# Another order for batch 0's attention and first products, and output products that wait for their low halves apart

## The chip, the cores and the metric

The kernel runs on one core of a Trainium2 chip. The metric is the device time of one execution in microseconds, measured over whole executions. The core's engines are called PE (TensorE, matmuls; PEld are its weight loads), DVE (VectorE), ACT (ScalarE), POOL (GpSimd) and SP (SyncE, which here only issues transfers).

## What is computed

Three stages follow each other on 4 batches of 768 tokens. All inputs are float32.

```python
# attention with decay: 8 heads, head_dim 48, state 48 x 48 per head
for t in range(S):
    state = alpha[:, :, t, :, None] * state + einsum('bhd,bhe->bhde', k[:, :, t], v[:, :, t])
    y[:, :, t] = einsum('bhd,bhde->bhe', q[:, :, t], state)
# x: the heads side by side, (4, 768, 384)
# first MLP with a spatial gate
h = gelu_tanh(x @ w_in)                       # 384 -> 1024
u, v = h[..., :512], h[..., 512:]
v_n = (v - mean(v)) / sqrt(var(v) + 1e-6) * g_ln
v_s = einsum('ts,bsd->btd', w_sg, v_n) + b_sg[None, :, None]
x = x + (u * v_s) @ w_out                     # 512 -> 384
# Fourier mixing and second MLP
u = x + real(fft(fft(x, axis=1), axis=2))
un = (u - mean(u)) / sqrt(var(u) + 1e-6)
out = u + relu(un @ w_ch1) @ w_ch2            # 384 -> 1536 -> 384
```

## The kernel before, in words

**Products in two halves.** A float32 product is made of three fp32r matmuls: each operand is split into a high half (written by ACT as a cast) and a low half (the rest, written by DVE as a difference), and PE adds high x high, high x low and low x high into one PSUM bank. `product(dst, terms)` (L1212 to L1219, its matmul is L1218) does this for a list of terms, in that order, term by term. Every matmul is preceded by its own weight load.

**How the program is written.** Each engine has its own queue of steps in an order written out by hand as lists of pairs ("step", index). Engines meet only through counting semaphores: a step waits until another engine's count is reached. An engine never goes past a step that waits.

**The opening (batch 0's attention and first products).** The lists `FIRST_DVE`, `FIRST_ACT`, `FIRST_POOL` and `FIRST_PE` (L73 to L96) order it. The tokens are six chunks (or tiles) of 128; the steps are:

- "prep" c and "query" c on DVE: two scans over the decays of chunk c (`rev` L953, `fwd` L965), each with a product into the decayed keys `kd` (L959) and queries `qu` (L969). The inputs of a chunk (`decay_k_q`) come by one transfer of 674 KB.
- "scores" c: PE transposes the keys (L1239) and multiplies keys by queries (L1251); DVE masks the result into `sm` (L983); ACT copies the keys by token into `kn` (L767).
- "out" c: PE makes the chunk's new state (L1273, for chunks 1 and 2 with the decayed state added by L1267) and its output (L1283, L1288); ACT copies the output to `y_by_token` (L770); for chunks 3 and 4 DVE keeps the state (L994) and "carry" decays it (L977); for chunks 1 to 3 "decay" on ACT does both (L781, L784).
- "x" t: PE transposes output tile t (L1320), ACT writes its high half `x_hi` (L797), DVE its low half `x_lo` (L1023).
- "v" t and "u" i: 6 products of 9 matmuls of 128x512 and 8 of 9 matmuls of 128x384 with the two halves of `w_in`. ACT applies the gelu (L803, L811). For v, DVE takes the statistics (L1032), POOL the reciprocal root `rs` (L649, L652), DVE normalizes (L999, "norm" below), ACT and DVE write the halves `vn_hi`, `vn_lo` (L790, L1004). "v" t on DVE also normalizes tile t-1 and writes the low half of tile t-2; "v end" does the last ones. v t needs the halves of x t and piece 0 of the weights, u i needs three tiles of x (0 to 2 for even i, all six for odd i) and piece 1.
- "next ..." are the first steps of batch 1's attention, made inside the opening.

`FIRST_PRODUCTS` is the order of u and v on PE. The products before index `FIRST_ROLLED`, and that one, all use bank 4, so each waits for the gelu of the one before; from `FIRST_ROLLED` + 1 on they roll over four banks, and wait until all of batch 0's attention is done (`wait_first_bank`, L1294 to L1303).

**The weight pieces.** The weights come as 12 pieces of 128x1536 in float32, through two raw buffers in the opening. Pieces 0 and 1 are `w_in`, 2 is `w_out`, 3 to 5 are `w_sg`. "split" n is ACT's high half (L755) and DVE's low half (L933). For pieces 2, 3 and 4 the low half is made otherwise: ACT writes the negated high half ("neg", L760) and POOL issues a transfer that adds the raw piece to it ("sum", L659). A piece's transfer (L526) is issued by SP when the piece before it in the same buffer has been read; SP's order is: chunks 0 to 3, pieces 0, 1, chunks 4, 5, pieces 2, 3, chunk 0 of batch 1, pieces 4, 5. Split 3 on ACT also waits for the whole of batch 0's attention, since `w_sg` lies over its buffers.

**The spatial stage.** After the opening, `phase1` runs for each batch: 8 spatial products s ("s" i, 18 matmuls of 128x384 with `w_sg`), each gated on DVE (L1063, L1067), split by ACT (`gated_hi`, L834) and DVE (`gated_lo`, L1009), and 8 output steps ("o" j, `output`, L1367 to L1378): three token tiles of 3 matmuls each with `w_out`, added up in three banks over four steps. The first spatial product of batch 0, `w_sg_hi` in the profile, waits for all halves of v, all gelus of u, and the low halves of pieces 2 to 5. The attention of the next batch runs beside it.

**The last stage.** `phase2` runs for each batch: 24 hidden steps "h" k (9 matmuls with `w_c1`; ACT writes `hidden_hi`, L885, DVE `hidden_lo`, L1165) and 24 output steps "o" k, each queued two hidden steps behind (`LAG = 2`), in two halves of 12 steps. An output step (L1480 to L1500) has 9 matmuls, 3 for each of three token tiles, into the banks `ACC`. After 12 steps "fin" on DVE adds each bank into `u_kept` (L1178) and counts `fin_done` once for each tile; the first output step of the next half waits for all three. The Fourier mixing of the next batch runs beside it.

## Time and profile before

| | |
|---|---|
| median of 3 runs (lowest, highest) | 710.98 us (709.78, 711.03) |
| the profiled execution | 710.78 us |
| its span, first to last instruction | 708.9 us |
| PE, PEld, DVE, ACT, POOL busy | 99%, 94%, 63%, 29%, 11% |
| mean granted TensorE clock | 0.998 |
| opening, to the first spatial product | 0 to 70.6 us |
| spatial stages of four batches | 70.6 to 376 us |
| last stage of four batches | 376 to 709 us |

The profiled execution's time is 1.9 us above its span: that is what lies around the first and the last instruction. All times inside the kernel are microseconds from the span's start. A matmul's listed duration overlaps the next one's, since they are pipelined; how fast PE goes is read from the distance of two starts. An idle time in brackets says how long the engine stood still before the instruction, and what ended it.

### The profile page before, as it was taken

What the parts mean: (1) busy time and instruction counts of PE and PEld (TensorE: products, weight loads), DVE (VectorE), ACT (ScalarE), POOL (GpSimd) and SP (SyncE); (2) the same over time, 40 slices, a digit from 0 to 9 for tenths busy, and PEclk for the clock granted to TensorE, in tenths of its full rate; (3) what the DMA queues carried; (4) which work ended last, traced back from release to release, by engine and by line L of the source; (5) the groups of instructions that cost most, each with busy time, mean ns of one, the idle gap of its engine ahead of it and who ended that gap; (6) DMA issues with size and microseconds to landing.
All of it is one profiled execution on the core that took longest, in us unless ns stands there. A gap on an engine that the chain in (4) does not pass through costs nothing.

```text
span 708.9 us, 13451 instructions
## 1 busy us (share of the span) xinstructions
PE 698.5 (99%) x5572; PEld 667.2 (94%) x5572; DVE 446.5 (63%) x859; ACT 204.3 (29%) x390; POOL 80.9 (11%) x125
## 2 busy tenths in 40 slices
PE   7999999999999999999999999999999999999998
PEld 6789999899998999989999999999999999999998
DVE  7997887996768967669587746381634726331212
ACT  2647111341114411144336222232221322222111
POOL 1022000120002100051211203001300201000000
PEclk9999999999999999999999999999999999999999
DMA  9757223322222131071346312012300200000000
GB/s 287 224 140 185 83 71 97 122 52 81 72 84 85 52 101 52 35 214 44 113 124 210 103 35 79 1 37 65 89 24 33 59 8 33 0 35 1 15 19 34
DMA packets 21358, 56.69 MB, mean 80 GB/s; under 512 B 2404, under 2 KB 14824, under 8 KB 21304
## 3 DMA queue, kind: packets, MB, share of 16 engines
q1 hardware_dynamic: 18104, 44.53, 20.3%
q0 software_dynamic: 3056, 11.26, 6.3%
q8 instruction: 40, 0.66, 0.4%
q10 hardware_dynamic: 144, 0.13, 0.1%
q14 instruction: 14, 0.11, 0.0%
HBM read 46.45 MB, written 9.46 MB: 79 GB/s over the span
## 4 chain that ended last, share of the span: by engine, by line
PE 92%; DVE 5%; DMA 2%; issue 1%; ACT 0%; SPq 0%; DVEq 0%; ACTq 0%
PE bank L1218 79%; PE bank L1251 3%; PE bank L1288 3%; PE bank L1283 2%; PE bank L1320 1%; PE bank L1438 1%; PE bank L1273 1%; PE bank L1239 1%; PE bank L1452 1%; DMA raw_weights_a<-in_w_second 1%; DVE u_kept L1178 1%; DMA decay_k_q<-in_akq 1%; DVE fwd L965 1%; DVE fwd_b L965 1%; DVE rev_b L953 1%
## 5 line engine op out<-in xcount | busy, mean ns | idle before, releaser
L1218 PE MATMUL bank<-ut_hi,w_c 128*128 128x384 f32 x576 | 162.8, 338 | 0.3 <-DVE hidden_lo L1165 0.3
L1165 DVE SCALAR_TENSOR_TENSOR hidden_lo<-bank,hidden_hi 128x384 fp32r<-128x384 f32 x96 | 53.4, 556 | 158.2 <-ACT hidden_hi L885 157.7
L1218 PEld LDWEIGHTS bank<-ut_hi,w_c 128*128 128x128 f32 x576 | 105.4, 188 | 1.2 <-DVE hidden_lo L1165 0.7
L885 ACT ACTIVATE hidden_hi<-bank 128x384 fp32r<-128x384 f32 x96 | 47.2, 492 | 199.5 <-PE bank L1218 199.2
L1218 PE MATMUL bank<-w_c_hi,hidden_hi 128*128 128x384 f32 x288 | 96.7, 336 | 0.5 <-DVE u_kept L1178 0.5
L1218 PE MATMUL bank<-ut_lo,w_c 128*128 128x384 f32 x288 | 96.3, 334 | 0.0
L1218 PE MATMUL bank<-w_c_hi,hidden_lo 128*128 128x384 f32 x288 | 96.3, 334 | 0.0
L1218 PE MATMUL bank<-w_c_lo,hidden_hi 128*128 128x384 f32 x288 | 96.2, 334 | 0.0
L1218 PE MATMUL bank<-w_sg_hi,vn_hi 128*128 128x384 f32 x192 | 66.2, 345 | 0.0
L1218 PE MATMUL bank<-w_sg_hi,vn_lo 128*128 128x384 f32 x192 | 64.2, 334 | 0.0
L1218 PE MATMUL bank<-w_sg_lo,vn_hi 128*128 128x384 f32 x192 | 64.2, 334 | 0.0
L834 ACT CAST gated_hi<-gated 128x384 fp32r<-128x384 f32 x32 | 16.4, 513 | 139.8 <-DVE gated L1067 139.8
L1218 PEld LDWEIGHTS bank<-w_c_hi,hidden_hi 128*128 128x128 f32 x288 | 54.1, 188 | 1.6 <-issue 1.6
L1218 PEld LDWEIGHTS bank<-ut_lo,w_c 128*128 128x128 f32 x288 | 54.2, 188 | 0.0
L1218 PEld LDWEIGHTS bank<-w_c_lo,hidden_hi 128*128 128x128 f32 x288 | 54.1, 188 | 0.0
L1218 PEld LDWEIGHTS bank<-w_c_hi,hidden_lo 128*128 128x128 f32 x288 | 54.1, 188 | 0.0
L1218 PEld LDWEIGHTS bank<-w_sg_hi,vn_hi 128*128 128x128 f32 x192 | 36.0, 188 | 1.6 <-issue 0.2
L1218 PEld LDWEIGHTS bank<-w_sg_lo,vn_hi 128*128 128x128 f32 x192 | 36.1, 188 | 0.0
L1218 PEld LDWEIGHTS bank<-w_sg_hi,vn_lo 128*128 128x128 f32 x192 | 36.0, 188 | 0.0
L1218 PE MATMUL bank<-w_out_hi,gated_hi 128*128 128x384 f32 x96 | 33.1, 345 | 0.4 <-DVE gated_lo L1009 0.4
L1218 PE MATMUL bank<-x_hi,w_in_hi 128*128 128x384 f32 x96 | 32.9, 342 | 0.0
L1218 PE MATMUL bank<-x_hi,w_in_lo 128*128 128x384 f32 x96 | 32.2, 335 | 0.0
(200 smaller groups left out, 1333.2 us busy)
## 6 DMA issues: line engine op xcount, KB each, us to landing
decay_k_q<-in_akq SPq DMA_DIRECT2D x19, 673.8 KB, 5.0
x_scratch<-x_half SPq DMA_DIRECT2D x8, 579.0 KB, 4.6
out_tiles<-u_kept SPq DMA_DIRECT2D x24, 192.0 KB, 2.0
values<-in_v SPq DMA_DIRECT2D x18, 192.0 KB, 5.1
x_quarters<-x_scratch SPq DMA_DIRECT2D x16, 168.9 KB, 3.2
raw_first_a<-in_w_first SPq DMA_DIRECT2D x3, 768.0 KB, 11.4
raw_first_b<-in_w_first SPq DMA_DIRECT2D x3, 768.0 KB, 4.7
raw_weights_b<-in_w_second SPq DMA_DIRECT2D x3, 768.0 KB, 5.3
```

The costliest lines, as they stand in the source:

```text
L834: nc.scalar.copy(gs[0][:, i % 3, :], gt[:, i % 3, :]).then_inc(ghi_done, 1)
L885: nc.scalar.activation(hid[0][:, i % 4, :], HB[i % 2][:, 0:HS], ACT.Relu).then_inc(hhi_done, 1)
L953: nc.vector.tensor_tensor_scan(rev[:, NA - 2::-1], raw[:, NA - 1:0:-1], resets[:, NA - 1:0:-1], 1.0, ALU.mult, ALU.add).then_inc(rev_done, 1)
L965: nc.vector.tensor_tensor_scan(fwd[:], raw[:, 0:NA], resets[:], 0.0, ALU.mult, ALU.add).then_inc(fwd_done, 1)
L1165: nc.vector.scalar_tensor_tensor(out=hid[1][:, i % 4, :], in0=HB[i % 2][:, 0:HS], scalar=0.0, in1=f32(hid[0][:, i % 4, :]), op0=ALU.max, o ...
L1178: nc.vector.tensor_tensor(ub[:, HT * i + j, :], ACC[j][:, 0:DM], ub[:, HT * i + j, :], ALU.add).then_inc(fin_done, 1)
L1218: ins = nc.tensor.matmul(dst, a, c, start=start and n == 0, stop=stop and n == len(passes) - 1)
L1239: ins = nc.tensor.transpose(ky[:, g * PR:(g + 1) * PR], kd[:, g, :], ident[0:PR, 0:PR])
L1251: ins = nc.tensor.matmul(sc[j][:, g * P:(g + 1) * P], kd[at, g, :], qu[at, g, :], start=True, stop=True)
L1273: ins = nc.tensor.matmul(sc[0][at, cols], kn[:, g, at], values[:, cols], start=not adds, stop=True, skip_group_check=True)
L1283: nc.tensor.matmul(ky[q, g * PP:(g + 1) * PP], qu[:, g, q], std[:, c % 2, g, :], start=True, stop=False, skip_group_check=True)
L1288: ins = nc.tensor.matmul(ky[q, h * D:(h + 1) * D], sm[:, g, j, q], values[:, h * D:(h + 1) * D], start=c == 0, stop=True, skip_group_check ...
```

## The change

It has two parts.

1. The four lists of the opening are written in another order, with `FIRST_ROLLED` at "v" 2 instead of "v" 3. No step is added or removed, and the code that carries the steps out is as it was. The pieces' transfers keep their places in SP's program; what they wait for (split 0, split 1, the high halves of pieces 2 and 3) stands elsewhere in the lists of ACT and DVE, and the sums of pieces 2 and 3 stand elsewhere in POOL's.
2. A new helper `tile_products` makes an output step of three token tiles: for each tile high x high and high x low of the weights, then a wait, then for each tile low x high. Before, the whole step waited for the low half of its operand; now it waits for the high half at its start (`ghi_done`, `hhi_done`) and for the low half before its last three matmuls (`glo_done`, `hlo_done`). It is used for the 32 output steps of the spatial stage and for the last stage's, but for the first of each half and the last two of all. The first output step of each half (f == 0) keeps the old order and waits for the sum of each tile by itself.

```diff
--- before.py
+++ after.py
@@ -71,28 +71,28 @@
 
 
 FIRST_DVE = ([("prep", 0), ("query", 0), ("prep", 1), ("scores", 0), ("query", 1), ("prep", 2)]
-             + [("scores", 1), ("query", 2), ("prep", 3), ("query", 3), ("scores", 2), ("split", 0)]
-             + [("x", 0), ("split", 1), ("scores", 3), ("prep", 4), ("x", 1), ("query", 4), ("out", 3)]
-             + [("x", 2), ("scores", 4), ("carry", 4), ("prep", 5), ("out", 4), ("query", 5), ("carry", 5)]
-             + [("v", 0), ("next prep", 0), ("x", 3), ("scores", 5), ("v", 1), ("x", 4), ("v", 2)]
-             + [("next query", 0), ("v", 3), ("x", 5), ("next scores", 0), ("v", 4), ("v", 5), ("split", 5)]
-             + [("v end", 0), ("v end", 1)])
-FIRST_ACT = ([("scores", 0), ("decay", 1), ("out", 0), ("scores", 1), ("scores", 2), ("decay", 2)]
-             + [("out", 1), ("scores", 3), ("split", 0), ("split", 1), ("x", 0), ("decay", 3), ("out", 2)]
-             + [("x", 1), ("split", 2), ("neg", 2), ("x", 2), ("v", 0), ("scores", 4), ("out", 3), ("x", 3)]
-             + [("u", 2), ("out", 4), ("v", 1), ("u", 4), ("scores", 5), ("x", 4), ("v", 2), ("out", 5)]
-             + [("split", 3), ("v", 3), ("neg", 3), ("next scores", 0), ("x", 5), ("split", 4), ("v", 4)]
-             + [("neg", 4), ("u", 6), ("v", 5), ("u", 0), ("split", 5), ("u", 3), ("u", 5), ("v end", 0)]
-             + [("u", 1), ("v end", 1), ("u", 7)])
-FIRST_POOL = ([("sum", 2), ("v", 0), ("v", 1), ("v", 2), ("sum", 3), ("v", 3), ("sum", 4), ("v", 4)]
+             + [("scores", 1), ("query", 2), ("x", 0), ("split", 0), ("prep", 3), ("scores", 2)]
+             + [("query", 3), ("split", 1), ("x", 1), ("prep", 4), ("scores", 3), ("query", 4), ("prep", 5)]
+             + [("x", 2), ("query", 5), ("out", 3), ("carry", 4), ("scores", 4), ("scores", 5), ("out", 4)]
+             + [("carry", 5), ("x", 3), ("v", 0), ("next prep", 0), ("x", 4), ("v", 1), ("next query", 0)]
+             + [("v", 2), ("x", 5), ("v", 3), ("v", 4), ("next scores", 0), ("v", 5), ("v end", 0)]
+             + [("v end", 1), ("split", 5)])
+FIRST_ACT = ([("scores", 0), ("out", 0), ("decay", 1), ("scores", 1), ("x", 0), ("split", 0)]
+             + [("decay", 2), ("out", 1), ("scores", 2), ("split", 1), ("v", 0), ("x", 1), ("scores", 3)]
+             + [("out", 2), ("split", 2), ("decay", 3), ("v", 1), ("x", 2), ("out", 3), ("scores", 4)]
+             + [("u", 4), ("neg", 2), ("u", 2), ("x", 3), ("scores", 5), ("out", 4), ("split", 3), ("x", 4)]
+             + [("out", 5), ("neg", 3), ("v", 2), ("split", 4), ("x", 5), ("v", 3), ("neg", 4), ("v", 4)]
+             + [("u", 0), ("v", 5), ("split", 5), ("u", 6), ("v end", 0), ("u", 7), ("v end", 1), ("u", 3)]
+             + [("next scores", 0), ("u", 5), ("u", 1)])
+FIRST_POOL = ([("v", 0), ("sum", 2), ("sum", 3), ("v", 1), ("v", 2), ("v", 3), ("sum", 4), ("v", 4)]
               + [("v", 5)])
-FIRST_PE = ([("scores", 0), ("out", 0), ("scores", 1), ("out", 1), ("scores", 2), ("scores", 3)]
-            + [("x", 0), ("out", 2), ("x", 1), ("v", 0), ("out", 3), ("x", 2), ("scores", 4), ("u", 2)]
-            + [("x", 3), ("out", 4), ("v", 1), ("scores", 5), ("u", 4), ("x", 4), ("v", 2), ("out", 5)]
-            + [("v", 3), ("x", 5), ("u", 6), ("next scores", 0), ("v", 4), ("u", 0), ("v", 5), ("u", 3)]
-            + [("u", 5), ("u", 1), ("u", 7)])
+FIRST_PE = ([("scores", 0), ("out", 0), ("x", 0), ("scores", 1), ("out", 1), ("scores", 2), ("v", 0)]
+            + [("x", 1), ("out", 2), ("scores", 3), ("v", 1), ("x", 2), ("out", 3), ("scores", 4)]
+            + [("u", 4), ("x", 3), ("scores", 5), ("u", 2), ("out", 4), ("out", 5), ("x", 4), ("v", 2)]
+            + [("v", 3), ("v", 4), ("x", 5), ("next scores", 0), ("v", 5), ("u", 0), ("u", 6), ("u", 7)]
+            + [("u", 3), ("u", 5), ("u", 1)])
 FIRST_PRODUCTS = [step for step in FIRST_PE if step[0] in ("u", "v")]
-FIRST_ROLLED = FIRST_PRODUCTS.index(("v", 3))
+FIRST_ROLLED = FIRST_PRODUCTS.index(("v", 2))
 FIRST_U = [i for step, i in FIRST_PRODUCTS if step == "u"]
 
 
@@ -1218,6 +1218,16 @@
                     ins = nc.tensor.matmul(dst, a, c, start=start and n == 0, stop=stop and n == len(passes) - 1)
                 return ins
 
+            def tile_products(dsts, x, w, lo_done, start, stop):
+
+                for dst, hi in zip(dsts, x[0]):
+                    nc.tensor.matmul(dst, hi, w[0], start=start, stop=False)
+                    nc.tensor.matmul(dst, hi, w[1], start=False, stop=False)
+                pe.wait_ge(*lo_done)
+                for dst, lo in zip(dsts, x[1]):
+                    ins = nc.tensor.matmul(dst, lo, w[0], start=False, stop=stop)
+                return ins
+
             def keep_warm(dst, times):
 
                 for _ in range(times):
@@ -1366,15 +1376,14 @@
 
             def output(b, j):
                 f = j % 4
-                pe.wait_ge(glo_done, 8 * b + j + 1)
+                pe.wait_ge(ghi_done, 8 * b + j + 1)
                 if j == 0:
                     pe.wait_ge(ug_done, 8 * (b + 1))
                 if j == 4:
                     pe.wait_ge(x1a_done, 2 * b + 1)
-                for t in range(HT):
-                    ins = product(GB[2 + t][:, 0:DM],
-                                  [([x[:, j % 3, t * P:(t + 1) * P] for x in gs],
-                                    [w[:, f, :] for w in w_out])], start=f == 0, stop=f == 3)
+                ins = tile_products([GB[2 + t][:, 0:DM] for t in range(HT)],
+                                    [[x[:, j % 3, t * P:(t + 1) * P] for t in range(HT)] for x in gs],
+                                    [w[:, f, :] for w in w_out], (glo_done, 8 * b + j + 1), f == 0, f == 3)
                 ins.then_inc(po_done, 1)
 
             def phase1(b, attends):
@@ -1479,24 +1488,31 @@
                             product(HB[i % 2][:, 0:HS], terms).then_inc(hid_done, 1)
                     elif step == "o":
                         h, f = i // NF, i % NF
-                        pe.wait_ge(hlo_done, 2 * NF * b + i + 1)
                         if f * DM % PIECE == 0 and isinstance(b, int) and b == 0:
                             wait_lo(pe, NP1 + KD + f * DM // PIECE)
                             pe.wait_ge(x1a_done, 2 * B)
-                        if f == 0:
-                            need(pe, fin_done, NT * b + HT * h)
                         if isinstance(b, int) and b == B - 1 and i >= 2 * NF - 2:
                             if i == 2 * NF - 1:
+                                pe.wait_ge(hlo_done, 2 * NF * b + i + 1)
                                 for j in range(HT):
                                     product(ACC[j][:, 0:DM],
                                             [([x[:, n % 4, j * P:(j + 1) * P] for x in hid],
                                               [w[:, n % NF, :] for w in w_c2]) for n in (i - 1, i)],
                                             start=False).then_inc(o_tile_done, 1)
                             continue
-                        for j in range(HT):
-                            ins = product(ACC[j][:, 0:DM],
-                                          [([x[:, i % 4, j * P:(j + 1) * P] for x in hid],
-                                            [w[:, f, :] for w in w_c2])], start=f == 0, stop=f == NF - 1)
+                        if f == 0:
+                            pe.wait_ge(hlo_done, 2 * NF * b + i + 1)
+                            for j in range(HT):
+                                need(pe, fin_done, NT * b + HT * (h - 1) + j + 1)
+                                ins = product(ACC[j][:, 0:DM],
+                                              [([x[:, i % 4, j * P:(j + 1) * P] for x in hid],
+                                                [w[:, f, :] for w in w_c2])], stop=False)
+                        else:
+                            pe.wait_ge(hhi_done, 2 * NF * b + i + 1)
+                            ins = tile_products([ACC[j][:, 0:DM] for j in range(HT)],
+                                                [[x[:, i % 4, j * P:(j + 1) * P] for j in range(HT)] for x in hid],
+                                                [w[:, f, :] for w in w_c2], (hlo_done, 2 * NF * b + i + 1), False,
+                                                f == NF - 1)
                         ins.then_inc(o_done, 1)
 
             pe.wait_ge(std_zeroed, 1)
```

## Rows read from the trace of the kernel before

**Rows 1.** Busy time by stretch: us, busy of each engine (instructions), PE clock, DMA, GB/s.

```profile
24.00:28.00 4.00, 4.00 (x41) 2.71 (x39) 3.52 (x5) 3.00 (x3) 0.00 (x0) 0.58 0.51 143
...
47.10:69.20 22.10, 22.10 (x166) 19.63 (x168) 17.26 (x37) 16.20 (x24) 6.91 (x12) 1.00 0.63 148
...
376.00:709.00 333.00, 329.11 (x2085) 324.98 (x2083) 147.32 (x295) 83.86 (x161) 32.44 (x40) 1.00 0.14 44
```

**Rows 2.** Timeline of DVE in the opening: start, us, engine, line, operation, out<-in.

```profile
19.46 0.06 DVE L950 MEMSET resets<- 112x4 f32 x1
...
25.28 1.76 DVE L933 TENSOR_TENSOR w_in_lo<-raw_first_a,w_in_hi 128x1536 fp32r<-128x1536 f32 x1 [0.48 <-ACT w_in_hi L755]
...
34.94 0.55 DVE L994 TENSOR_TENSOR state<-bank,state_decayed 112x384 f32<-112x384 f32 x1
...
35.40 0.55 DVE L1023 TENSOR_TENSOR x_lo<-bank,x_hi 128x384 fp32r<-128x384 f32 x1
...
38.25 0.06 DVE L950 MEMSET resets<- 112x4 f32 x1
...
40.22 0.55 DVE L994 TENSOR_TENSOR state<-bank,state_decayed 112x384 f32<-112x384 f32 x1
...
46.36 0.55 DVE L1023 TENSOR_TENSOR x_lo<-bank,x_hi 128x384 fp32r<-128x384 f32 x1
```

**Rows 3.** Timeline of PE in the opening.

```profile
34.59 0.55 PE L1239 MATMUL bank<-constants,kd 112*128 112x112 f32 x4
...
36.17 0.44 PE L1218 MATMUL bank<-x_hi,w_in_hi 128*128 128x384 f32 x1
...
37.85 0.49 PE L1320 MATMUL bank<-constants,y_by_token_even 128*128 128x128 f32 x3
...
38.27 0.56 PE L1273 MATMUL bank<-values_first,kn 128*48 128x48 f32 x16
...
40.37 0.50 PE L1218 MATMUL bank<-w_in_hi,x_hi 128*128 128x512 f32 x1
...
47.06 0.52 PE L1320 MATMUL bank<-constants,y_by_token_even 128*128 128x128 f32 x3 [1.11 <-DVE x_lo L1023]
...
70.58 0.44 PE L1218 MATMUL bank<-w_sg_hi,vn_hi 128*128 128x384 f32 x1
```

**Rows 4.** What PE waited for: us in total, times, longest.

```profile
PE bank L1218 <- DVE u_kept L1178: 0.5, 3, 0.2
```

**Rows 5.** Timeline of PE and DVE between two halves of the last stage.

```profile
508.87 0.33 PE L1218 MATMUL bank<-w_c_hi,hidden_lo 128*128 128x384 f32 x1
509.05 0.33 PE L1218 MATMUL bank<-ut_hi,w_c 128*128 128x384 f32 x1
...
509.31 1.49 DVE L1178 TENSOR_TENSOR u_kept<-bank,u_kept 128x384 f32<-128x384 f32 x3 [0.55 <-PE bank L1218]
...
510.43 0.34 PE L1218 MATMUL bank<-ut_hi,w_c 128*128 128x384 f32 x1
510.95 0.41 PE L1218 MATMUL bank<-w_c_hi,hidden_hi 128*128 128x384 f32 x1 [0.18 <-DVE u_kept L1178]
511.20 0.33 PE L1218 MATMUL bank<-w_c_lo,hidden_hi 128*128 128x384 f32 x1
```

**Rows 6.** Timeline of PE and ACT at output steps and at the last stage's start.

```profile
124.31 0.44 PE L1218 MATMUL bank<-w_out_hi,gated_hi 128*128 128x384 f32 x1 [0.18 <-DVE gated_lo L1009]
...
373.80 0.44 PE L1218 MATMUL bank<-w_out_hi,gated_hi 128*128 128x384 f32 x1 [0.22 <-DVE gated_lo L1009]
...
377.26 1.48 ACT L755 CAST w_c_hi<-raw_weights_a 128x1536 fp32r<-128x1536 f32 x1 [2.73 <-DMA raw_weights_a<-in_w_second]
...
379.77 0.44 PE L1218 MATMUL bank<-ut_hi,w_c 128*128 128x384 f32 x1 [0.34 <-DVE hidden_lo L1165]
```

**Rows 7.** Instructions on `w_sg_lo`, 61 to 63 us: sum 4's issue and landing.

```profile
L659 POOL DMA_DIRECT2D w_sg_lo<-in_w_first x1: 883/883/883, 62.1 to 62.1; - x1
...
DMA to landing us min/median/max: 7.6/7.6/7.6
```

## The prediction

> **What bounds the kernel now.** I read the busy table by stretch first, then the two timelines of the opening batch, then the waits of TensorE (PE). From 47 us on PE is the bound: it is busy 22.10 of the 22.10 us up to 69.20, and 329.11 of the last 333 us, at a granted clock of 1.00 [rows 1]. Ahead of that VectorE (DVE) is the bound: between 19.46 and 35.40 us its steps stand end to end with one idle spell of 0.48 us [rows 2]. PE's last long wait there is 1.11 us, for DVE's `x_lo` of token tile 3, and from 47.06 us it runs unbroken to the first spatial product at 70.58 us [rows 3]. So time is won in two ways only: reach the point from which PE never waits with less PE work left, or take away the few waits that PE still has behind it. The granted clock was 0.58 in 24 to 28 us [rows 1], but DVE was late there anyway.
>
> **Part one, the order of batch 0.** No instruction is added or removed; every queue gets its steps in another order, and the last PE wait moves. Below, "x2" is tile 2 of the transposed input, "v" and "u" the two halves of the first product, "s0" the first spatial product.
>
> DVE, up to its step x2. Before, its twelve steps behind query 2 (prep 3, query 3, scores 2, split 0, x0, split 1, scores 3, prep 4, x1, query 4, out 3, x2) start at 19.46, and x2 starts at 35.40 [rows 2]. The new list has the same steps ahead of x2, without out 3 (35.40 - 34.94 = 0.46) and with prep 5 (40.22 - 38.25 = 1.97) [rows 2]. Without the 0.48 of idle, x2 starts at 19.46 + 15.94 - 0.48 - 0.46 + 1.97 = 36.43. I keep the 0.48 out because the steps around split 0 changed places: its input is now asked for after x0, when ScalarE (ACT) has long had time to split the piece. Were it to come back, everything is 0.5 later; that is my first uncertainty.
>
> PE, from u4. In the new PE list u4 is the first product that waits for x2. Ahead of it stands scores 4, which waits for DVE's query 4, done when prep 5 begins, at 36.43 - 1.97 = 34.46; its matmuls end some 1.2 later, so PE idles about 1.4 us, until u4. In the trace PE restarted 0.70 us after such an `x_lo` began (46.36 to 47.06) [rows 2, 3], so u4 starts at 37.13. What is left from there to s0 is the old list from x4 to s0, 70.58 - 47.06 = 23.52 us, with the same fourteen steps in another order, and five more: u4 and u2 at 37.85 - 36.17 = 1.68 each, x3 at 0.42, scores 5 at 36.17 - 34.59 = 1.58, out 4 at 40.37 - 38.27 = 2.10 [rows 3]. That is 7.46, so s0 starts at 37.13 + 23.52 + 7.46 = 68.11, which is 2.47 earlier. Where does this come from? The stall is 9.93 us earlier and only 7.46 us of work more stands behind it: v0, v1 and x1 have gone into holes through which PE used to idle, between 20 and 31 us.
>
> What this needs; its times are estimates, added up queue by queue from the steps' durations in the timelines that the rows are from. (a) Scores 5 waits for the state that DVE's out 3 writes: DVE is through query 5 and out 3 near 39.6, PE gets there at 39.7: no slack, no loss. (b) Out 5 waits for carry 5, near 44.3 against 44.4. (c) v3 needs the bank of out 5's copy, and ACT now has split 3 (a 1.5 us cast that waits for out 5) and x4 ahead of that copy: it ends near 48.5, when PE wants it. I take 0.1 for these and bound them at 0.8. (d) DVE must be done with its whole list before s0; adding its steps up it ends near 66.7, 1.4 ahead. Nothing of this is lost later if PE stays the bound, and to 125 us it does. I take **2.4**, between 1.0 (0.5 of idle back, 0.8 of small waits) and 3.0 (half a microsecond of restarts inside the 23.52 that the new order may not have; nothing in the rows gives more).
>
> The transfers. SyncE's and GpSimd's own programs are changed only in the place of `sum` 2 and 3. Piece 2 is asked for when split 0 is done, some 5 us earlier, piece 5 when split 3's first half is, some 5 us earlier too; pieces 3 and 4 hardly move. Chunks 4 and 5 were queued ahead of piece 2 on the same queue and are needed by DVE 3 to 6 us after they landed, so I cost this at nothing. Sum 2 goes behind rs 0 on GpSimd, some 12 us later, and sum 3 ahead of rs 1, which DVE wants only by norm 1; each issue holds GpSimd for 0.9. Sum 4 decides: it was issued at 62.1 and landed 7.6 later [rows 7]. On ACT its negation stands behind out 5 (read at 46.0), split 3, x4, out 5's copy, neg 3, v2, split 4, x5 and v3: with 1.48 for each cast or negation of a piece [rows 6], 0.4 to 0.5 for a tile and 1.0 for a v, and x5's input there at 53.4, it ends near 56.7. Its issue is near 57.2, so it lands at 64.8, 3.3 ahead of s0.
>
> **Part two, output products that wait by parts.** The nine matmuls of an output step are the same, in another order (six that need only the high halves, then three), with one more wait in the middle. 32 steps of the spatial stage and 86 of the last stage take it.
> A satisfied wait costs nothing in these rows: across the border from an output step to a hidden one, where a wait stands, starts are 0.18 apart (508.87, 509.05), no more than inside a product [rows 5]. So 118 more of them cost nothing if they are met, and in the last stage they are: the low half is asked for two hidden products after it was made.
> The first product of each half now waits for the sum of each tile by itself. PE stood idle for it 3 times, 0.5 in total [rows 4]. The true price is larger: 510.43 to 510.95 is 0.52 and the next distance 0.25, where 0.18 is usual: 0.41 each [rows 5]. DVE starts the three sums at 509.31, 0.5 apiece, so the first is done at 509.9, and PE wants it at 510.61 [rows 5]. All three go: 1.2; by idle time alone 0.5.
> Of the two waits for `gated_lo`, the one at 124.31 (0.18 idle) goes, since the high half is written 0.6 earlier: 0.2. The one at 373.80 goes too, but buys nothing: the next stall, at 379.77, waits for `hidden_lo`, and ahead of that on ACT stands a cast of a weight piece that waited for its transfer until 377.26 [rows 6]. PE comes there earlier and waits longer. So part two is **1.4**, between 0.5 and 2.2 (with what 373.80 and its restart cost, kept).
>
> Here stands the one rule against the change. Rows: an output step already goes through three banks, and the last stage had 1.00 throughout [rows 1, 5]. The Trainium skill, TensorE: Matmul & The Clock Gate, section on a second HAM failure mode, psum-queue depth-cycling, tells of a kernel whose clock fell again and again because it cycled through PSUM banks at each iteration; the new order changes banks more often. By the rows the sum stays; by the rule it is a rival below.
>
> **Sum.** 2.4 + 1.4 = 3.8. The profiled execution took 710.78, so it would be 706.98; the median of the runs shown is 710.98, 0.2 above it. I say **707.1**. Its own range is 705.8 (3.0 + 2.2) to 709.5 (1.0 + 0.5).
>
> **The rivals.** About 0.2% of this time, 1.4 us, is what a measurement can tell from no change: faster ends at 709.6, slower begins at 712.4.
> *The summed pieces come late.* For: sums 2 and 3 and piece 5 now share the transfer engines between 47 and 60 us, so sum 4 finds a queue; against: it has 3.3 us of room. If its landing takes 12 instead of 7.6, s0 starts at 69.2 and 1.1 is lost: 708.2. 0.13.
> *The won time is given back.* s0 is earlier, but DVE, with little slack for rs and norm of v4 and v5, ends its list later than I add up, or batch 1's first chunks do. Only part two is left: 709.6. Against: DVE is busy 17.26 of the 22.10 us before s0 [rows 1], so it has room. 0.10.
> *It doesn't do what it says:* the pieces move only by their waits, and small waits (a) to (c) eat the rest: 710.5. 0.04.
> *Slower: the wait in the middle breaks the stream.* PE's first start after a real wait costs 0.07 more than usual (0.25 against 0.18) [rows 5]. If each new wait did that even when met, because the weights of the seventh matmul aren't fetched ahead of it, 118 x 0.07 = 8.3: 707.1 + 8.3 = 715.4. It decides from 0.05 per wait. Against it: the step borders above, with waits and without loss. 0.06.
> *Slower: banks and clock.* If changing banks brought the granted clock down to the 0.58 of 24 to 28 us [rows 1] in the 118 steps, 1.6 us each (nine times 0.18) would take 2.8: 142 more, 849. Against: three banks in turn at 1.00 already. This is what the Trainium skill's rule above would do here, and no row shows it. 0.01.
>
> **How the numbers follow.** The forecast has 0.66. The range is 705.6 to 709.6: it takes in the first two rivals, and leaves out no change and slower (0.11) and the tails. Faster: 0.66, most of the first rival, half of the second: 0.80. Same: the rest of those and "doesn't do": 0.13. Slower: 0.07.
>
> **What would show it.** Right: a PE wait for `x_lo` of 1 to 1.5 us ending near 37.1 and no longer one up to s0; s0 (first `w_sg_hi`) near 68.1; no PE wait for `u_kept`; starts 0.17 apart through the middle of an output step; the stall of 379.77 some 0.4 longer. Wrong: s0 starting on a transfer landing, or after DVE's last split; PE waits between 37 and 55 that add up to over 1 us; distances of 0.25 at each seventh matmul; clock under 1.00 in the last stage.

## The result and the profile after

The changed kernel takes 705.97 us (median of four runs, 705.21 to 706.89), the kernel before took 710.44 beside it (709.78 to 711.03, four runs). The ratio is 0.9938 with a 95% interval of 0.9926 to 0.9949: faster by 4.5 us. The forecast was 707.1 in a range from 705.6 to 709.6. The profiled execution took 705.21, with a span of 703.4; it is the lowest of the four. One execution of the kernel before, in a later experiment, took 1746.73 us for a reason that nothing on record shows, and the ratios leave it out.

The table of busy time by stretch, columns as in [rows 1]. The first stretch is the same 4 us; the other two are moved to where their work now stands:

```profile
24.00:28.00 4.00, 3.93 (x76) 2.96 (x76) 3.93 (x6) 1.00 (x3) 0.00 (x0) 1.00 0.97 321
47.00:67.50 20.50, 20.50 (x154) 18.34 (x152) 18.14 (x38) 16.08 (x25) 10.16 (x14) 1.00 0.85 198
376.00:704.00 328.00, 324.43 (x2064) 321.62 (x2062) 144.37 (x290) 81.88 (x159) 31.82 (x39) 1.00 0.13 40
```

PE is busy throughout the second stretch, as in [rows 1], and the transfer engines work 0.85 of it where they worked 0.63. In 24 to 28 us PE now executes 76 matmuls instead of 41, and the transfer engines are at 0.97 instead of 0.51.

The timeline of PE around its last wait of the opening and at the first spatial product, against [rows 3]:

```profile
32.95 0.39 PE L1293 MATMUL bank<-state_decayed,qu_b 112*64 112x96 f32 x4 [0.65 <-ACT state_decayed L784]
...
35.22 1.16 PE L1261 MATMUL bank<-qu,kd 48*128 48x128 f32 x16
36.85 0.41 PE L1218 MATMUL bank<-x_hi,w_in_hi 128*128 128x384 f32 x1 [0.47 <-issue]
...
67.82 0.44 PE L1218 MATMUL bank<-w_sg_hi,vn_hi 128*128 128x384 f32 x1
```

And of DVE, against [rows 2]: the step x2 and the end of the list.

```profile
36.20 0.55 DVE L1023 TENSOR_TENSOR x_lo<-bank,x_hi 128x384 fp32r<-128x384 f32 x1
...
64.64 1.75 DVE L933 TENSOR_TENSOR w_sg_lo<-raw_first_b,w_sg_hi 128x1536 fp32r<-128x1536 f32 x1
66.34 0.06 DVE L950 MEMSET resets<- 112x4 f32 x1
```

The first spatial product came at 67.82 instead of 70.58. PE idled 0.47 us ahead of u4 and 0.65 ahead of out 3, which waited for ACT's decayed state.

```profile
30.40 1.48 ACT L755 CAST w_out_hi<-raw_first_a 128x1536 fp32r<-128x1536 f32 x1 [1.51 <-DMA raw_first_a<-in_w_first]
31.78 1.03 ACT L784 ACTIVATE state_decayed<-bank,rev_b 112x96 f32<-112x96 f32 x4
```

That is ACT's timeline in the opening: the decay stands behind the cast of weight piece 2, and the cast waited 1.51 us for the piece's transfer. The piece was asked for at 21.58, which is 5.5 us earlier than before (27.07), but landed only 0.9 earlier (30.37 instead of 31.23): it took 8.8 us instead of 4.2.

The instructions on `w_sg_lo` from 56 to 60 us, which answer to [rows 7]:

```profile
L659 POOL DMA_DIRECT2D w_sg_lo<-in_w_first x1: 873/873/873, 57.0 to 57.0; - x1
...
DMA to landing us min/median/max: 10.1/10.1/10.1
```

Sum 4 went out at 57.0 and landed 10.1 later, at 67.1, only 0.7 ahead of the first spatial product.

The table of PE's waits, in full; of those in [rows 4] and [rows 6] none is left:

```profile
PE bank L1239 <- DVE state_decayed L1181: 1.7, 1, 1.7
PE bank L1261 <- DVE qu L969: 0.7, 1, 0.7
PE bank L1249 <- DVE kd L959: 0.7, 1, 0.7
PE bank L1293 <- ACT state_decayed L784: 0.6, 1, 0.6
PE bank L1330 <- ACT y_by_token_even L770: 0.6, 1, 0.6
PE bank L1218 <- issue: 0.5, 1, 0.5
PE bank L1283 <- DVE sm L983: 0.2, 1, 0.2
```

The timeline between two halves of the last stage, against [rows 5]. L1228 is the product of the low half in the new function `tile_products`, L1224 and L1225 are those of the high half.

```profile
505.05 1.49 DVE L1178 TENSOR_TENSOR u_kept<-bank,u_kept 128x384 f32<-128x384 f32 x3 [0.55 <-PE bank L1228]
...
506.17 0.33 PE L1218 MATMUL bank<-ut_hi,w_c 128*128 128x384 f32 x1
506.34 0.33 PE L1218 MATMUL bank<-w_c_hi,hidden_hi 128*128 128x384 f32 x1
506.51 0.33 PE L1218 MATMUL bank<-w_c_lo,hidden_hi 128*128 128x384 f32 x1
```

The second half's first output product starts 0.17 behind the product before it, and the next again 0.17 behind: the distances of 0.52 and 0.25 of [rows 5] are gone.

Last, the timeline of PE and ACT at the output steps and at the last stage's start, against [rows 6]:

```profile
121.30 0.44 PE L1224 MATMUL bank<-w_out_hi,gated_hi 128*128 128x384 f32 x1
...
372.58 1.48 ACT L755 CAST w_c_hi<-raw_weights_a 128x1536 fp32r<-128x1536 f32 x1 [1.15 <-DMA raw_weights_a<-in_w_second]
```

The wait at 124.31 is gone, and so is the stall at 379.77, which I had expected to grow. The reason shows in ACT's row: weight piece 9 landed 4.2 us after its issue here and 5.8 after it in the profile before, so ACT waited 1.15 instead of 2.73.

**Where the 5.6 us between the two profiles are.** I cut both at the same instructions: the first spatial product, the first of batch 1, the first of batch 3, the first hidden product, the last matmul.

| stretch | before | after | gain |
|---|---|---|---|
| start to first spatial product | 70.58 | 67.82 | 2.76 |
| batch 0's spatial stage, to batch 1's | 93.00 | 92.75 | 0.25 |
| to batch 3's spatial stage | 165.29 | 165.20 | 0.09 |
| to the first hidden product | 47.17 | 46.71 | 0.46 |
| last stage | 329.61 | 327.61 | 2.00 |

That is more than the medians differ by (4.5), since the profile of after is of its quickest run, and that of before is 0.3 above its median. How much of it belongs to the change and how much to how early a transfer happened to land is what the experiments had to settle.

### The profile page after: what moved, and what is told of

It reads as the page before. It is cut to its first block, busy times and chain, and to the rows that moved or that the text cites. A ratio compares the mean times of both kernels' runs of the same rounds, so it can differ in the third digit from the quotient of the medians.

```text
span 703.4 us, 13455 instructions
## 1 busy us (share of the span) xinstructions
PE 695.0 (99%) x5572; PEld 666.3 (95%) x5572; DVE 446.3 (63%) x859; ACT 204.3 (29%) x390; POOL 81.6 (12%) x125
## 4 chain that ended last, share of the span: by engine, by line
PE 95%; DMA 2%; DVE 2%; issue 1%; ACT 0%; SPq 0%; DVEq 0%
PE bank L1218 55%; PE bank L1224 9%; PE bank L1228 9%; PE bank L1225 9%; PE bank L1261 3%; PE bank L1298 3%; PE bank L1293 2%; DMA raw_first_a<-in_w_first 1%; PE bank L1447 1%; PE bank L1283 1%; PE bank L1461 1%; PE bank L1249 1%; PE bank L1330 1%; DMA decay_k_q<-in_akq 1%; DVE fwd L965 0%
## 5 line engine op out<-in xcount | busy, mean ns | idle before, releaser
L1224 PE MATMUL bank<-w_c_hi,hidden_hi 128*128 128x384 f32 x258 | 86.3, 335 | 0.0
L1225 PE MATMUL bank<-w_c_lo,hidden_hi 128*128 128x384 f32 x258 | 86.2, 334 | 0.0
L1228 PE MATMUL bank<-w_c_hi,hidden_lo 128*128 128x384 f32 x258 | 58.6, 334 | 0.0
L1225 PEld LDWEIGHTS bank<-w_c_lo,hidden_hi 128*128 128x128 f32 x258 | 48.4, 188 | 0.0
L1224 PEld LDWEIGHTS bank<-w_c_hi,hidden_hi 128*128 128x128 f32 x258 | 48.4, 188 | 0.0
L1228 PEld LDWEIGHTS bank<-w_c_hi,hidden_lo 128*128 128x128 f32 x258 | 46.0, 188 | 0.0
L1224 PE MATMUL bank<-w_out_hi,gated_hi 128*128 128x384 f32 x96 | 33.1, 345 | 0.0
```

Source lines behind the costliest of these rows:

```text
L1224: nc.tensor.matmul(dst, hi, w[0], start=start, stop=False)
L1225: nc.tensor.matmul(dst, hi, w[1], start=False, stop=False)
L1228: ins = nc.tensor.matmul(dst, lo, w[0], start=False, stop=stop)
```

## The experiments

In each, "before" is the unchanged earlier kernel, run on the same chip among the others. Its median was 710.62, 711.49 and 710.71 us in the three groups of experiments, so kernels of different groups are compared by their ratios and not by their medians.

### One part at a time

`lists_alone` is the kernel before with the new lists of batch 0 and nothing else; `parts_alone` is the changed kernel with the old lists. The diff between `parts_alone` and the change:

```diff
-FIRST_DVE = (... ("query", 3), ("scores", 2), ("split", 0), ... ("out", 3), ("x", 2) ...)
+FIRST_DVE = (... ("query", 4), ("prep", 5), ("x", 2), ("query", 5), ("out", 3) ...)
 (and FIRST_ACT, FIRST_POOL, FIRST_PE and FIRST_ROLLED in the same way)
```

> The new lists of the opening without the waits by parts. Mine: the first spatial product at 67.8 us as in the changed kernel (70.58 before), and nothing of this is lost later: 2.8 us less than before, and the three waits for u_kept of 0.18 each and the wait for gated_lo in the first spatial stage still there. Rival (the opening's gain is given back in the first spatial stage, where DVE is busy): first spatial product at 67.8, but the last stage begins less than 2 us earlier than before, and the time is 1 us or more above mine.

> The waits by parts (and the sums waited for tile by tile) with the old lists. Mine: 1.2 us for the three waits for u_kept, 0.2 to 0.7 for gated_lo: 1.4 to 1.9 us less than before, first spatial product unchanged at 70.6. Rival (the two parts need each other, so alone this gives nothing): within 0.5 us of before. Rival (a wait in the middle costs 0.07 us even when met): 8 us slower with the sums left out.

Measured: `lists_alone` 707.74 us (six runs, 706.92 to 708.45), ratio 0.9954, interval 0.9940 to 0.9967. `parts_alone` 708.55 (twelve runs, 707.50 to 711.25), ratio 0.9970, 0.9956 to 0.9983. Before was 710.62. So 2.9 and 2.1 us, 5.0 added up, where the change itself brings 4.9 (next experiment): within what the intervals allow, about 1 us either way, the two parts add up.

In the profile of `lists_alone` the first spatial product starts at 67.76, in that of `parts_alone` at 70.62. The opening's gain is the lists' alone. In the timeline of PE in `lists_alone` the old wait between the halves is still there, along with another:

```profile
359.00 0.41 PE L1218 MATMUL bank<-w_out_hi,gated_hi 128*128 128x384 f32 x1 [0.70 <-DVE x_half L1017]
...
508.17 0.41 PE L1218 MATMUL bank<-w_c_hi,hidden_hi 128*128 128x384 f32 x1 [0.18 <-DVE u_kept L1178]
```

Its last stage takes 328.87. The one at 359 goes back to the residual rows of batch 3, which land late in some executions and early in others: DVE waited 1.82 us for them at 346.92, and 0.49 at the same step of the changed kernel. It turns up again below.

### The two kernels once more

`after_again` and `before_again` are unchanged, to see what differs between executions of one program.

> The changed kernel once more, beside the two above. Mine: the two parts add up, so its gain is that of lists_alone plus that of parts_alone within 0.4 us, 4.2 to 4.7 us. Its executions fall on two levels about 1.2 us apart, and the slower ones are those in which the weight piece read by the first cast of w_c_hi lands 5 to 6 us after its issue instead of 4.2, so that PE waits for hidden_lo in the last stage's third hidden product. Rival: they overlap, the sum is over 1 us more than the whole.

> The kernel before once more, for a second profile. Mine: by stretches it is 70.6 to the first spatial product, 93.0 and 165.2 to the fourth batch's, 46.7 to 48.1 to the last stage (more where the mirrored residual rows land late), and 328.8 plus up to 1.0 for the last stage (more where the piece of w_c_hi lands over 4.6 us after its issue). So the opening does not vary in the old order by more than 0.2, and all of the spread sits in the last two. Rival: the opening varies as in the new order.

Measured: `after_again` 705.77 (eight runs, 705.03 to 710.87), ratio 0.9936, 0.9915 to 0.9957. The highest had a mean granted clock of 0.993, and there is no profile of it; the other seven, at 0.999 or 1.000, end at 707.21. The profile has the same last stage (327.57, piece 9 landed after 4.2), and is still 0.8 above the other one: the first spatial product came at 68.16 instead of 67.82, and batch 3 has a wait of 0.40 for `x_half`. So the "two levels from piece 9" are not the whole of it.

The 0.34 in the opening has two parts. DVE is 0.2 later from its first steps on (x2 at 36.41 instead of 36.20). And PE came to u4 without a wait, later still, since piece 2 landed at 31.35 and ACT's decay 3 stands behind its cast; the timelines of ACT and PE:

```profile
31.38 1.48 ACT L755 CAST w_out_hi<-raw_first_a 128x1536 fp32r<-128x1536 f32 x1 [1.65 <-DMA raw_first_a<-in_w_first]
...
33.93 0.39 PE L1293 MATMUL bank<-state_decayed,qu_b 112*64 112x96 f32 x4 [0.93 <-ACT state_decayed L784]
```

PE had also waited 0.73 for `values_first`, the second part of batch 0's values, at 25.25, but it idled 0.93 behind that, so this wait cost nothing here.

`before_again` 710.61 (eight runs), ratio 1.0007 (0.9992 to 1.0021): first spatial product at 70.66, last stage 328.85, with piece 9 landing after 4.2 and no stall at the place of 379.77. Its table by stretch has this for 24 to 28 us:

```profile
24.00:28.00 4.00, 4.00 (x85) 3.32 (x83) 3.53 (x5) 4.00 (x7) 0.00 (x0) 1.00 0.64 172
```

A granted clock of 1.00 where [rows 1] had 0.58, and the first spatial product at the same time to 0.1. (PE had waited 1.05 and about 0.35 in the 2 us ahead in both profiles.) The low clock in the profile of before cost nothing: DVE was the bound there.

### Is the wait in the middle free, and the change of banks?

`waits_x5` repeats the wait that `tile_products` has in its middle five times; `banks_in_turn` goes through the three banks twice, changing at every matmul.

```diff
-                pe.wait_ge(*lo_done)
+                for _ in range(5):
+                    pe.wait_ge(*lo_done)
```

```diff
-                for dst, hi in zip(dsts, x[0]):
-                    nc.tensor.matmul(dst, hi, w[0], start=start, stop=False)
-                    nc.tensor.matmul(dst, hi, w[1], start=False, stop=False)
+                for n in range(2):
+                    for dst, hi in zip(dsts, x[0]):
+                        nc.tensor.matmul(dst, hi, w[n], start=start and n == 0, stop=False)
```

> The changed kernel with the wait for the low half written five times over in each of the 118 output steps that have it in the middle. Mine (a wait that is met costs PE nothing): starts 0.17 to 0.18 us apart through the middle of a step, time within 0.4 us of the changed kernel. Rival (each wait costs PE some of its stream, hidden so far by one wait's slack): 472 more waits at 0.07 us are 33 us; at 0.02 us still 9.

> The changed kernel with the six high matmuls of such a step in the order of the weights' halves, so that every matmul goes to another bank than the one before it. Mine (changing banks costs nothing): same starts, same granted clock of 1.00, within 0.4 us of the changed kernel. Rival (cycling through banks makes the clock fall, as the Trainium skill's page TensorE: Matmul & The Clock Gate tells under psum-queue depth-cycling): granted clock under 1.00 in the last stage and 5 us or more slower.

Measured: `waits_x5` 706.37 (four runs, 704.88 to 708.00), ratio 0.9917, 0.9893 to 0.9941; `banks_in_turn` 706.06 (four runs, 705.85 to 707.24), ratio 0.9919, 0.9896 to 0.9941. The two stand within 0.3 of each other. The timeline of PE in `waits_x5`, one output step of the last stage (L1224 and L1225 the high half, L1229 the low half behind the five waits):

```profile
395.71 0.33 PE L1224 MATMUL bank<-w_c_hi,hidden_hi 128*128 128x384 f32 x1
...
396.57 0.33 PE L1225 MATMUL bank<-w_c_lo,hidden_hi 128*128 128x384 f32 x1
396.75 0.68 PE L1229 MATMUL bank<-w_c_hi,hidden_lo 128*128 128x384 f32 x3
397.27 0.33 PE L1218 MATMUL bank<-ut_hi,w_c 128*128 128x384 f32 x1
```

Across the five waits the distance is 0.18, and the whole step takes 1.56, nine times 0.173. Its last stage takes 327.57, to the hundredth what `after_again` took. A met wait on PE costs nothing that can be seen here, not even five in a row at 118 places (32 of them in the spatial stages, whose stretches are unchanged too, 92.75 to batch 1): the rival that priced them at 8.3 us is refuted.

The same in `banks_in_turn`, and below it that kernel's table by stretch:

```profile
394.94 0.68 PE L1225 MATMUL bank<-w_c_hi,hidden_hi 128*128 128x384 f32 x3
395.46 0.68 PE L1225 MATMUL bank<-w_c_lo,hidden_hi 128*128 128x384 f32 x3
395.98 0.68 PE L1228 MATMUL bank<-w_c_hi,hidden_lo 128*128 128x384 f32 x3
396.50 0.33 PE L1218 MATMUL bank<-ut_hi,w_c 128*128 128x384 f32 x1
```

```profile
376.00:705.00 329.00, 325.39 (x2067) 322.15 (x2065) 145.68 (x291) 82.86 (x161) 32.07 (x39) 1.00 0.13 41
```

0.52 for three, and a granted clock of 1.00 over the whole stage. The Trainium skill, TensorE: Matmul & The Clock Gate, section on a second HAM failure mode, psum-queue depth-cycling, tells of a clock that fell again and again in a bf16 kernel with N = 512, which cycled through PSUM banks at each iteration and idled shortly between its groups of matmuls. This trace doesn't show it: with float32 matmuls of 128x384 and no idle time between the steps, another bank at every matmul left the clock at 1.00.

The profile of `waits_x5` has a surprise at quite another place, the opening. First spatial product at 70.61; PE's timeline and the table by stretch say why:

```profile
27.33 0.78 PE L1278 MATMUL bank<-state_decayed,constants 112*112 112x384 f32 x1 [2.14 <-DMA values_first<-in_v]
```

```profile
24.00:28.00 4.00, 1.86 (x9) 1.03 (x7) 3.93 (x7) 0.97 (x2) 0.00 (x0) 0.95 1.04 241
28.00:32.00 4.00, 4.00 (x68) 3.27 (x67) 3.79 (x5) 0.00 (x0) 0.00 (x0) 0.63 0.97 319
```

PE waited 2.14 us for the second part of batch 0's values, and in the 4 us that follow the granted clock was 0.63. The opening's gain is all gone in this execution, the slowest of the four. The edit is not what did it: the step has no `tile_products` in it, `after_again` waited 0.73 at this place, and the median is as good as that of the others. DVE's timeline shows how a wait of PE gets to x2: DVE's scores 3 reads PE's product of that chunk, and x2 stands behind it.

```profile
33.53 1.29 DVE L983 TENSOR_TENSOR sm_b<-bank,constants 128x512 f32<-128x512 f32 x2 [1.66 <-PE bank L1262]
```

Of the 2.8 that the first spatial product is later than in the profile of after, 1.66 is this. Another 0.87 was there before PE waited at all (x1 on DVE at 29.30 instead of 28.43), since chunks 0 and 1 too had landed late.

### Hiding the cast of piece 9

The stall at 379.77 hung on ACT, which casts piece 9 and only then makes the first hidden tiles. `split9_behind_hidden` puts the cast behind the first hidden tile.

```diff
-              ("end", 0): [("turn", 4), ("turn", 5), ("split hi", 9)]}
+              ("end", 0): [("turn", 4), ("turn", 5)]}
...
-    if i in SPLIT_IN_P2 and isinstance(b, int) and b == 0 and SPLIT_IN_P2[i][0] == "split":
+    if i in SPLIT_IN_P2 and isinstance(b, int) and b == 0:
```

> The changed kernel with ACT's cast of w_c_hi (piece 9) moved behind the first hidden_hi. Mine (the two levels come from that transfer, because the first hidden_hi is queued behind the cast that waits for it): no PE wait for hidden_lo at the last stage's start, and only the faster level, so the median is 0.3 to 0.7 us below the changed kernel's. Rival (the two levels have another cause, such as the span's start or the clock): medians within 0.2 us, both levels seen again.

Measured: 705.98 (six runs, 705.80 to 707.24), ratio 0.9933, 0.9920 to 0.9947. A miss: no quicker than `after_again` in the same group. The stall is not gone but changed its name; PE's timeline:

```profile
378.01 0.44 PE L1218 MATMUL bank<-w_c_hi,hidden_hi 128*128 128x384 f32 x1 [0.62 <-DVE w_c_lo L933]
```

PE now waits for the split piece itself, which the first output product needs. The last stage took 328.50 with piece 9 landing after 4.9, where `better_order` with the same landing took 327.85. So the edit made a stall of its own: the piece landed at 373.18, but ACT, now busy with the first hidden tile, began its cast at 374.69, and the first output product needs the piece. With the landing at 4.2 the changed kernel has no stall in either place, but the transfer can't be issued earlier in this program: its buffer lies over the halves of v, and it waits for the last spatial product.

### Does PE's last wait set the first spatial product?

`x2_later` changes two neighbours in DVE's list, so that x2 comes behind query 5.

```diff
-             + [("x", 2), ("query", 5), ("out", 3), ("carry", 4), ...
+             + [("query", 5), ("x", 2), ("out", 3), ("carry", 4), ...
```

> The changed kernel with DVE's x2 moved behind query 5 (2.1 us of work). Mine (u4, the first product that waits for x2, starts the stretch in which PE never waits): u4 starts near 38.9 instead of 36.85, scores 5 no longer waits, the first spatial product near 69.8, 2.0 us slower than the changed kernel. Rival (the opening's end is set by transfers or by DVE's list): first spatial product still at 67.8 to 68.2, same time.

Measured: 709.27 (eight runs, 707.21 to 712.46), ratio 0.9963, 0.9943 to 0.9983. u4 starts at 38.87, 0.65 behind x2 on DVE, as in the changed kernel and in four others, and as expected; but the first spatial product starts at 71.06, not at 69.8. PE's timeline and the table by stretch:

```profile
38.87 0.66 PE L1218 MATMUL bank<-x_hi,w_in_hi 128*128 128x384 f32 x1 [2.63 <-issue]
39.32 0.52 PE L1218 MATMUL bank<-x_lo,w_in_hi 128*128 128x384 f32 x1
39.64 0.52 PE L1218 MATMUL bank<-x_hi,w_in_lo 128*128 128x384 f32 x1
...
41.88 0.38 PE L1330 MATMUL bank<-constants,y_by_token_even 128*128 128x128 f32 x2
```

```profile
38.80:41.90 3.10, 3.04 (x10) 2.97 (x11) 2.42 (x5) 0.00 (x0) 0.00 (x0) 0.50 0.58 224
```

After 2.63 us of idling, u4's matmuls stand 0.32 apart instead of 0.17, at a granted clock of 0.50, that is 1.2 GHz. They take 3.01 from 38.87 to 41.88, and 1.67 in the changed kernel's profile (36.85 to 38.52): 1.3 lost, and the distance from 69.8 to 71.06 is 1.3. So the mechanism holds, 2.02 later at u4 is 2.0 later at the first spatial product, and the long idle spell has a price of its own on top. Piece 9 landed after 5.8 here, as in the profile before, and its last stage took 328.78.

`better_order` goes the other way: x2 ahead of prep 5 on DVE, and decay 3 ahead of the cast of piece 2 on ACT.

```diff
-   FIRST_DVE: ... ("query", 4), ("prep", 5), ("x", 2), ("query", 5) ...
+   FIRST_DVE: ... ("query", 4), ("x", 2), ("prep", 5), ("query", 5) ...
-   FIRST_ACT: ("split", 2), ("decay", 3) ... ("u", 4), ("neg", 2), ("u", 2), ("x", 3) ...
+   FIRST_ACT: ("decay", 3), ("split", 2) ... ("u", 4), ("x", 3), ("u", 2) ... ("neg", 2) ...
-   FIRST_PE:  ("x", 3), ("scores", 5), ("u", 2)
+   FIRST_PE:  ("x", 3), ("u", 2), ("scores", 5)
```

> The changed kernel with DVE's x2 ahead of prep 5, ACT's decay 3 ahead of split 2, PE's u2 ahead of scores 5, ACT's neg 2 behind out 4. By my theory of the stall u4 starts near 35.4 (1.4 earlier), but scores 5, out 4 and out 5 are then late on DVE's prep 5, query 5 and carry 5, so only 0.2 to 0.8 of it reaches the first spatial product: 67.0 to 67.6, where sum 4 (it landed at 67.1 in the changed kernel's profile) may hold it. Rival (PE's own work sets the end once u4 is earlier): first spatial product at 66.4.

Measured: 705.57 (six runs, 704.84 to 708.54), ratio 0.9920, 0.9898 to 0.9942. A miss in the profile: u4 starts at 36.27 where I expected 35.4, and without a wait, 1.9 behind x2 on DVE. So x2 no longer sets it but the work that PE has ahead of it, which a wait of 0.87 for `values_first` had made late. The first spatial product came at 68.11. Whether it is quicker than the change by a few tenths can't be told from these runs.

### What makes `values_first` late?

GpSimd issues that transfer when chunk 2 of batch 0 has landed, and right behind it three more small ones. `bias_later` keeps these back until the values are there; `bias_later_better` is the same on `better_order`.

```diff
-            pool.wait_ge(akq_in[3], 16)
+            pool.wait_ge(val_first_in[1], 16)
             pool.dma_start(g_col[:], g_ln).then_inc(vectors_in, 16)
```

> The changed kernel with the transfers of b_sg, g_ln and the row table issued when the last four chunks of values have landed, not beside them (they are needed 40 us later). Mine (in the new order out 2 on PE waits for values_first; it landed at 24.4 to 24.9 in most profiles and over 26 in one, where PE idled 2.1 us there, its clock fell and the first spatial product came at 70.6): values_first lands up to 1 us earlier, no PE wait for it over 0.3 us, first spatial product at 67.7 to 67.9, median 0 to 0.4 us below the changed kernel's and no execution above 708. Rival (the queue ahead of the values sets their landing): landing and spread as before.

> The same edit in better_order. Mine: its first spatial product came at 68.1 with a wait of 0.9 for the values; without it 67.2 to 67.6, so 705.0 to 705.4. Rival (sum 4's landing at 67.1 to 67.5 or DVE's list holds it): 67.8, same time as the changed kernel.

Measured: 706.23 (six runs, 704.80 to 708.76), ratio 0.9930, 0.9914 to 0.9946; and 705.76 (six runs, 704.92 to 708.01), ratio 0.9933, 0.9916 to 0.9949. The theory that the small transfers take the values' turn fell. GpSimd's row in `bias_later`:

```profile
13.49 0.94 POOL L639 DMA_DIRECT2D values_first<-in_v  x1 [12.63 <-DMA decay_k_q_c<-in_akq]
```

With nothing behind it on GpSimd's queue, the transfer still landed 13.3 us after its issue, at 26.8, and PE waited 2.28 for it. In the thirteen other profiles it took 12.1 to 13.0 from issue to landing, so what differs more is the issue, which hangs on chunk 2's landing: 12.3 in the profile of after, 12.8 in `after_again`, 14.4 in `waits_x5`. PE takes these values with its products at L1277 (L1267 in the kernel before). With the new lists it started them on the landing itself, in the profile of after at 24.42 for 12.3 + 12.1 = 24.4, in `after_again` at 25.25. With the old ones it came at 26.11 in the profile of before and at 25.24 in `before_again`, where the values had landed at 24.6 and 25.0, and in `parts_alone` just as they landed, at 25.18. So the new order has brought PE to the values 0.8 us or more earlier, and used up the little room there was.

In the profile of `bias_later_better` PE waited 0.46 at this place, for DVE, and the first spatial product came at 67.53, as expected (67.2 to 67.6); the median of 705.76 is above the 705.0 to 705.4 that I had expected. Beside it, the 0.87 of waiting in `better_order` cost up to 0.6.

### Does the first spatial product start on sum 4?

`sum4_last` sends sum 4 behind rs 5 on GpSimd.

```diff
-FIRST_POOL = ([..., ("v", 3), ("sum", 4), ("v", 4)] + [("v", 5)])
+FIRST_POOL = ([..., ("v", 3), ("v", 4)] + [("v", 5), ("sum", 4)])
```

> The changed kernel with GpSimd's sum 4 behind the last v instead of ahead of v4. It tests the rival of my forecast in which the summed pieces set the end of the opening. Mine: issue near 62.8 instead of 57.0, landing 7.6 to 10 later, at 70.4 to 72.8, and PE's first spatial product waits exactly for it: 2.6 to 5 us slower. If the first spatial product stays at 67.8, nothing there depends on that transfer.

Measured: 708.52 (eight runs, 706.76 to 711.17), ratio 0.9962, 0.9951 to 0.9972. The instructions on `w_sg_lo`, and PE's timeline:

```profile
L659 POOL DMA_DIRECT2D w_sg_lo<-in_w_first x1: 871/871/871, 62.7 to 62.7; - x1
...
DMA to landing us min/median/max: 6.9/6.9/6.9
```

```profile
69.91 0.41 PE L1218 MATMUL bank<-w_sg_hi,vn_hi 128*128 128x384 f32 x1 [2.08 <-DMA w_sg_lo<-in_w_first]
70.16 0.46 PE L1218 MATMUL bank<-w_sg_lo,vn_hi 128*128 128x384 f32 x1
...
71.38 0.52 PE L1218 MATMUL bank<-w_sg_hi,vn_lo 128*128 128x384 f32 x1
```

Issued at 62.7, landed at 69.6, and the product starts at 69.91: the rival "the summed pieces come late", made on purpose. The landing took less than the 7.6 to 10 us that I had expected, and so the product is 2.1 later than in the profile of after and not 2.6 or more. Behind a wait of 2.08 the matmuls are again 0.32 apart. In the changed kernel the landing at 67.1 leaves 0.7, so the rival was closer than I had it.

## Why the prediction was right, and where not

**The result.** 705.97 against 707.1; inside the range of the forecast itself. The mechanism of both parts is what the runs show: the opening's end moves with x2 (`x2_later`), and each part alone brings its share. The sum forecast was 3.8, the medians give 4.5 and 4.9. Term by term:

**Part one: 2.4, measured 2.76** in the profile, 2.9 by the medians of `lists_alone`. Of the working, the long term held to the hundredth: from u4 to the first spatial product 23.52 + 7.46 = 30.98 was the forecast, and 30.97 was measured (36.85 to 67.82). So the counting of "the old list from x4 on, and five steps more" was sound, and the 0.1 for small waits wasn't needed. The miss is in DVE's sum: x2 started at 36.20, not at 36.43, and u4 at 36.85, not at 37.13. Half of it, 0.12, is only that DVE began its next step behind query 2 at 19.34 here and at 19.46 in the profile before, and `after_again`, at 19.54, has it the other way. The 0.48 of idle, the first uncertainty, did not come back.

**The idle before u4** I put at 1.4 us; it was 0.47. Here a step was left out. I took scores 4 on PE from DVE's query 4 alone, but PE was itself held up, 0.65 for ACT's decay 3, which stood behind a cast that waited for piece 2. The error had no effect on u4's start, which DVE sets in this profile; in `after_again` the same step held PE for 0.93 and made u4 some 0.2 later. Whether the forecast's own idle time of 1.4 would have brought the clock down no run shows: waits of 0.73 to 0.93 didn't, and 2.63 did, at 1.3 on top of itself.

**Sum 4's landing** was mis-sized: 7.6 us from [rows 7], 10.1 measured, so a room of 0.7 instead of 3.3. The issue was forecast well (57.2 against 57.0). Outside the first rival I had costed the crowding of the pieces' transfers at nothing, though I had them all between 47 and 60; the share of 0.85 in that stretch is what it looks like. No time was lost by it, and `sum4_last` shows that it would be as soon as it lands behind 67.8.

**The transfers, "cost nothing"**, is the step that failed in kind, in two places. Piece 2, asked for 5.5 us earlier, took 8.8 us instead of 4.2 and held decay 3 up; that cost nothing in the profile of after and some 0.2 in `after_again`. And I asked only whether the moved pieces would be late, and not whether PE, with v0 and x1 brought forward into its idle time, would reach an unmoved transfer sooner. It does, for the second part of the values: in the profiled execution it cost next to nothing, in others PE waits 0.2 to 2.3 us. The nine profiles with the new lists in which DVE's x2 and sum 4 stand as the change has them, or earlier, have the first spatial product between 67.53 and 70.61; the three with the old lists have it between 70.58 and 70.66. Waits up to 0.73 cost nothing (0.57 in `split9_behind_hidden` has 67.79), as PE waits further on anyway, and 0.87 cost up to 0.6 in `better_order`, where it doesn't. Waits above 2 us cost most of the gain: 70.14 in `bias_later`, where DVE stood 1.82 for PE at scores 3, and 70.61 in `waits_x5`, where 0.87 of it was DVE's own lateness. PE's slow spell of about 3 us behind the wait is in these figures too. All of this is read from profiles; no run held chunk 2 back on purpose.

**Part two: 1.4, measured 2.0** by stretches (0.25 + 0.46 + 1.26) and 2.1 by the medians of `parts_alone`. Its first term was 1.2 for three waits of 0.41. Kernels with the old wait for `u_kept` and no stall for piece 9 (landing after 4.2 and 4.8) took 328.85 and 328.87 for the last stage, those with the new one and a landing after 4.2 took 327.57 to 327.61: 1.26. Idle time alone would have said 0.5; reading the distance between starts was right. The term of 0.2 at 124.31 measured 0.25. The third is the one that I set at nothing: the wait at 373.80 goes, worth 0.46 (47.17 to 46.71), and I said that the stall at 379.77 gives it back. That depends on when piece 9 lands, which I had taken as fixed from one profile. The last stage of kernels with the new waits:

| piece 9's landing, us after its issue | last stage, us | kernel |
|---|---|---|
| 4.2 | 327.57 | `after_again`, `waits_x5` |
| 4.3 | 327.59 | `bias_later_better` |
| 4.8 | 327.78 | `bias_later` |
| 4.9 | 327.85 | `better_order` |
| 5.3 | 328.22 | `parts_alone` |
| 5.7 | 328.65 | `sum4_last` |
| 5.8 | 328.78 | `x2_later` |
| 6.1 | 329.04 | `banks_in_turn` |

At 5.8, as in the profile of before, the forecast step holds. The profile of before had 329.61, which is 327.57 + 1.26 + 0.78 of stall and restart; `x2_later` has 327.57 + 1.21. The stall grew by 0.43 and gave back what 373.80 had won. At 4.2 there is no stall to give it to, and the 0.46 stays. The profile of before had met a late landing, its other one (`before_again`) an early one, so 0.74 of the 2.00 in the table of stretches is the landing's and not the change's. Nor is the 0.09 between batches 1 and 3, a stretch that took 165.17 in `before_again`. That leaves 2.76 + 0.25 + 0.46 + 1.26 = 4.7, which agrees with the medians' 4.5 and 4.9.

**The rivals.** Waits in the middle: refuted by `waits_x5`. Banks and clock: refuted by `banks_in_turn`. The summed pieces late: not in this kernel, real in `sum4_last`. The won time given back at DVE's list: DVE's list ended at 66.34, against 66.7 in the forecast, and the stretch to batch 1 lost nothing (92.75). Doesn't do what it says: refuted by `lists_alone`.

**Open** stays why the same transfer lands after 4.2 us in one execution and after 6.1 in another, what happened in the execution at a mean clock of 0.993, and whether `better_order` is worth its few tenths. No version ran that clearly beats the changed kernel.

## What to carry to other kernels

Count what stands between the last wait and the point where the bound engine runs unbroken: with PE as the bound behind it, moving that wait 10 us forward and putting 7.5 us more of work behind it gave the difference, to 0.3 us. Take a wait's price from the distance between starts (0.41), not from its idle time (0.18), and split a wait wherever the parts come ready one after another, since a met wait cost nothing. And before costing a stall that ends on a transfer, look at how that landing varies: one profile is one draw, here between 4.2 and 6.1 us, and a new order may take away the room that hid it.
